# Placing the heads' products one product earlier in each step of a fused attention and mixture-of-experts kernel

## What is computed

```python
# q, k, v: (8, 8, 576, 64), float32: batch, heads, sequence, head dimension
kv = np.einsum('bhsd,bhse->bhde', k, v)
out = np.einsum('bhsd,bhde->bhse', q, kv)
rms = np.sqrt(np.mean(out * out, axis=-1, keepdims=True) + 1e-06)
x = out / rms * g_norm            # then laid out as 4608 tokens x 512

gate = 1.0 / (1.0 + np.exp(-(x @ w_gate)))   # 512 x 1536
x = gate * (x @ w_val) @ w_out               # 1536 x 512

h = x @ w_in                                 # 512 x 2048
g = where(h >= 1, h, where(h <= -1, 0, (h + 1) ** 2 / 4))
y = g @ w_out                                # 2048 x 512
```

## Time and profile before

| | |
|---|---|
| median of three runs | 1758.91 us (1757.97 to 1762.51) |
| the profiled execution, its own time | 1760.77 us |
| its span, from first to last instruction | 1759.0 us |
| TensorE matmul busy | 1680.4 us (96%) |
| VectorE busy | 1215.1 us (69%) |
| ScalarE busy | 886.3 us (50%) |
| GpSimd busy | 227.4 us (13%) |
| mean granted TensorE clock | 0.981 |

### The profile page before, as it was taken

The page is one execution under the profiler, slowest core; times in us unless marked ns, Lnnn a source line. Parts: engine busy times, 40 slices in busy tenths (PEclk is TensorE's granted clock), DMA queues, the critical chain, the costliest instruction groups (busy, mean ns, idle before and its releaser), DMA issues. The chain is left out here.

```text
span 1759.0 us, 31916 instructions
## 1 busy us (share of the span) xinstructions
PE 1680.4 (96%) x12552; PEld 1641.2 (93%) x12552; DVE 1215.1 (69%) x1725; ACT 886.3 (50%) x1612; POOL 227.4 (13%) x293
## 2 busy tenths in 40 slices
PE   8999999999879999899999899999995799999999
PEld 5799999999879999899999899999995799999999
DVE  4567677678657775787778777777773576667764
ACT  5556666655435554444445455555552344444443
POOL 3510000014333442100002500000001100000000
PEclk9999999999989999999999999999997999999999
DMA  7444443333777788944533423333338944434440
GB/s 255 136 144 132 143 145 128 104 127 126 196 198 217 211 238 258 301 142 147 151 131 137 142 104 129 130 130 130 135 135 276 304 140 128 125 120 145 143 121 37
DMA packets 229316, 278.90 MB, mean 159 GB/s; under 512 B 33072, under 2 KB 172848, under 8 KB 229168
## 3 DMA queue, kind: packets, MB, share of 16 engines
q1 hardware_dynamic: 191568, 207.66, 36.0%
q0 software_dynamic: 37600, 69.22, 13.4%
HBM read 156.76 MB, written 120.06 MB: 157 GB/s over the span
## 5 line engine op out<-in xcount | busy, mean ns | idle before, releaser
L1500 PE MATMUL x<-t_hi,v_lo 128*128 128x288 f32 x1664 | 501.3, 301 | 34.7 <-ACT kept L877 19.0
L1501 PE MATMUL x<-t_lo,v_hi 128*128 128x288 f32 x1664 | 495.2, 298 | 0.0
L1502 PE MATMUL x<-t_hi,v_hi 128*128 128x288 f32 x1664 | 494.0, 297 | 0.0
L1500 PEld LDWEIGHTS x<-t_hi,v_lo 128*128 128x128 f32 x1664 | 316.1, 190 | 42.1 <-ACT kept L877 21.2
L1502 PEld LDWEIGHTS x<-t_hi,v_hi 128*128 128x128 f32 x1664 | 317.3, 191 | 0.0
L1501 PEld LDWEIGHTS x<-t_lo,v_hi 128*128 128x128 f32 x1664 | 316.7, 190 | 0.1
L1500 PE MATMUL y<-t_hi,v_lo 128*128 128x288 f32 x832 | 250.9, 302 | 26.3 <-DVE c_tile L1054 19.6
L1501 PE MATMUL y<-t_lo,v_hi 128*128 128x288 f32 x832 | 247.5, 297 | 0.0
L1502 PE MATMUL y<-t_hi,v_hi 128*128 128x288 f32 x832 | 246.7, 296 | 0.0
L1500 PEld LDWEIGHTS y<-t_hi,v_lo 128*128 128x128 f32 x832 | 158.1, 190 | 32.5 <-DVE c_tile L1054 20.0
L1500 PE MATMUL x<-v_hi,t_lo 128*128 128x256 f32 x576 | 164.2, 285 | 8.7 <-ACT o_kept L1021 8.7
(11 more groups left out here) (195 smaller groups left out, 3647.4 us busy)
## 6 DMA issues: line engine op xcount, KB each, us to landing
g_scratch<-c_tile SPq DMA_DIRECT2D x128, 288.0 KB, 2.4
gq<-g_scratch SPq DMA_DIRECT2D x64, 512.0 KB, 6.2
h_scratch<-gate SPq DMA_DIRECT2D x192, 144.0 KB, 2.1
hq<-h_scratch SPq DMA_DIRECT2D x32, 864.0 KB, 5.1
stage<-w_in POOLq DMA_DIRECT2D x68, 256.0 KB, 3.3
kv_ring<-kv_in SPq DMA_DIRECT2D x30, 512.0 KB, 4.4
fold_hi<-fold_hi POOLq DMA_DIRECT2D x14, 896.0 KB, 5.4
fold_lo<-stage POOLq DMA_DIRECT2D x14, 896.0 KB, 7.4
```

The costliest lines, as they stand in the source:

```text
L1500: nc.tensor.matmul(dst, s_lo, m_hi, start=start, stop=False, skip_group_check=True)
L1501: nc.tensor.matmul(dst, s_hi, m_lo, start=False, stop=False, skip_group_check=True)
L1502: return nc.tensor.matmul(dst, s_hi, m_hi, start=False, stop=stop, skip_group_check=True)
```

## The change

The call of `heads` inside `attention` is made at P4's place in place of P6's. `attention(k, 4)` is called behind P4 of step k - 1, which stands directly ahead of P6 of step k, so the six matmuls of the heads move ahead of the six matmuls of P6 in 24 steps. Nothing else differs.

```diff
             def attention(k, number):
 
                 b, s = divmod(k, A_SETS)
-                if number == 6 and heads_of(k):
+                if number == 4 and heads_of(k):
                     heads(*heads_of(k))
```

## The result

| | before | after |
|---|---|---|
| median | 1759.06 us | 1777.75 us (1776.40 to 1780.12, four runs) |
| span of the profiled execution | 1759.0 us | 1776.8 us |
| TensorE matmul busy | 1680.4 us (96%) | 1684.9 us (95%) |
| VectorE busy | 1215.1 us | 1213.2 us |
| ScalarE busy | 886.3 us | 882.8 us |

The ratio is 1.0104, with a 95% interval of 1.0086 to 1.0123: 18 us slower, where 1777.0 was forecast. No engine has more work; TensorE waits.

A forecast was written before the change was run, and what follows sets the result against it. TensorE was taken to bound the heads' stretch. Five regular groups, 16.1 us, with the first group made 18.1; added to the 1758.91 median this gave 1777.0 us, own range 1774 to 1780, 8-in-10 range 1767 to 1781.

The forecast's parts named there:

- TensorE alone bounds the stretch: Over 85 to 370 us TensorE is busy 283.61 of 285.00 us, so every new wait adds its full length.
- The squares hang on P6, not on the heads: On ScalarE the squares follow P6's copy and the casts back to back, so moving P6 back delays them.
- the first rival: Only what was already late counts, so the mean square's new wait is absent: 8 to 9 us, 1767.5; chance 0.13.
- 0.72 at s = 5: In steps with two casts, TensorE's mean square waits 0.72 us for `ps_lo`, which was 0.08 early before.
- 0.62 for the heads at s = 0: At s = 0 the heads can start at 7.45 for a place at 6.83, waiting 0.62 us for `pq_lo`.
- A regular group 3.2: Each of five regular groups of four heads steps loses 3.2 us in waits and restarts, 16.1 in all.
- 0 at k = 4 in the first group: The heads fill P6's 0.91 wait, but a weight chunk's low part holds the next P1: 0, largest gain 0.8.
- What stays hidden: P7, P4, P6 and P3 still get the copies and `c` they need before their places, so no wait there.
- The longer-chain rival: Lateness of `pq_lo` reaches into the next step's cast: 4.2 to 4.5 us a group, 1783 to 1785; chance 0.09.
- The rule on VectorE's drain: If each next VectorE operation awaited an empty pipe, five distances grow 0.08, about 1.1 us a group; forecast went by rows instead.
- Not given back: Later passes just start later; the rival, chance 0.05, had the loss recovered at 470 to 480 us's folded-weight wait: 1758.9.
- the prediction's own signs of being wrong: A ScalarE gap between the casts and `ps_hi`, no wait of the mean square, or shorter passes behind.

The follow-up runs named there:

- The half at s = 4 and 5: Against the kernel before, the heads move ahead of P6 only at s = 4 and 5 (12 of 24 steps): 1766.63 us, ratio 1.0048.
- the half at s = 5 and 1: Against the kernel before, the heads move ahead of P6 only at s = 5 and s = 1: 1764.93 us, ratio 1.0024.
- the rearranged kernel: The change plus squares and high part ahead of ScalarE's copy behind P6, and `pq_lo` and `ps_lo` earlier on VectorE: 1762.80 us, 1.0022 against the kernel before.

## Why the prediction was right

By its own steps:

- *TensorE alone bounds the stretch, so every new wait counts in full.* Right: 18.3 us inside, 17.8 on the span, 18 by the ratio.
- *The squares hang on P6, not on the heads.* Right, and the point on which the first rival fell. The half at s = 4 and 5, the half at s = 5 and 1, and the squares moved ahead on ScalarE each gave what this predicts to within 0.2 us inside. The rival's 8 to 9 us for the whole change would have been 1767.5.
- *0.72 at s = 5.* Measured, from the group shown: the heads start at 195.12 and the mean square at 200.66, 5.54 later, less 4.79 for the heads, P6, P3, P2, P7 and P1: 0.75.
- *0.62 for the heads at s = 0.* From the mean square (200.66) to the heads (203.40) 2.74, less the 2.12 of the earlier trace rows: 0.62.
- *A regular group 3.2.* Measured, from group to group: 50.39 less 47.13, 3.26. Five groups and what the first has behind its first mean square make 18.3; expected were 5 x 3.2 and 2.0, 18.1.
- *0 at k = 4 in the first group.* Right. This step lies ahead of the first mean square and so outside the inside distance, and the executions differed by then: at its very first loads TensorE had waited 1.36 us in the kernel after and 0.62 in the kernel before. From a matmul of `x` that both traces show behind a short wait ahead of k = 4 (69.10 before, 70.19 after) to the first mean square (91.13 and 92.22) it is 22.03 us in both. The first heads wait 0.42 for `pq_lo`, P6 no longer waits its 0.91, and the next P1 waits 0.73 for the low part of a weight chunk (0.25 before).
- *What stays hidden.* Right: no wait for the copies behind P1, P6 or P7 has appeared in the stretch.
- *The longer-chain rival.* It fell: a group cost 3.26, not 4.2 to 4.5.
- *The rule on VectorE's drain.* The instructions behind `ps_lo` followed one another as in the earlier trace rows, 0.68, 0.37 and 0.67 apart. The prediction says that such rows contradict the Trainium skill ("VectorE: DVE Perf Modes", The DRAIN you can't avoid); that is too strong, since the same paragraph goes on: "A next op that is not held starts earlier". Both kinds stand in the traces: at s = 4 of the rearranged kernel `c` started only 0.03 behind the end of `pq_lo`, in all six groups, and cost the 0.1 a group named above. There it is the first instruction to read PSUM behind the copies of `kv_raw`, which take half of the partitions each; directly behind these copies it had also started 0.03 behind the end in the kernel before. Whether that is the cause was not tested.
- *Not given back.* Right in the main: the execution ends 17.8 us later, and of the 18.3 nothing came back where the rival had it, at the waits for folded weights. Over 265 us from 460 (before) and from 480 (after) TensorE waited 17.9 and 20.9 us for ScalarE's copy of line 877, which stands there behind casts of folded weights; in the four experiments with that line it was 17.4 to 19.3. But one of the prediction's own signs of being wrong, passes behind that are shorter than before, did appear: from the last mean square to the end it was 1759.0 - 348.2 = 1410.8 us and is 1776.8 - 367.6 = 1409.2. The sign was badly chosen, since this distance lies between 1405.6 and 1410.8 in the eight profiled executions, and the kernel before has the longest of them. The 17.8 of the spans is near 18.3 in part by chance: the start had added 1.1 and the passes behind took 1.6 away, as told in the last section.
- *How the waits would show.* I expected 16 or 17 waits of the mean square and about 6 us; the profile lists 13 and 6.9. The waits of 0.14 are not listed; the 13 are the first mean square's and one behind each s = 5 and s = 0.

## What to carry to other kernels

When work moves within the list of the engine that bounds, look on the other engines not for who uses its result, but for what stands ahead of that user in its list: here the squares could start only behind a copy that the move had pushed back, and an input that had come 0.08 us early came 0.72 late. Move the followers' lists together with it, or leave it. And judge a wait by taking away its cause: to move only the instruction that waits shifts the same lateness to the next place that needs the chain.

## What the runs showed beside this

In the profiled executions the clock behind a wait far from the change was not the same each time. Behind the end of the second product, TensorE waited 2.80 us in the kernel before and 1.87 in the one after (the wait of line 1009), and in six microseconds that begin 2.2 to 2.5 us behind it the granted clock was 0.74 and 1.00. The windows of the kernel before:

```profile
1016.00:1022.00 6.00, 6.00 (x36) 6.00 (x36) 4.10 (x7) 2.81 (x5) 0.00 (x0) 0.74 0.27 101
```

and of the kernel after:

```profile
1036.00:1042.00 6.00, 6.00 (x48) 6.00 (x47) 5.31 (x8) 3.32 (x7) 0.00 (x0) 1.00 0.26 101
```

48 matmuls in place of 36 in the same six microseconds: the lower level (1.2 GHz in place of 2.4) cost the kernel before about 1.6 us there (12 matmuls at 0.13), and its longer wait another 0.9. A start that was 19.4 us late at the last mean square (18.3 and 1.1 from the start of the execution) and 21.1 us at the end of the second product was so 18.6 us late behind this stretch. Another 0.9 went at the wait for `c_tile` (line 1054), 18.12 us in the kernel before, near 1358 us, and 17.24 in the kernel after, near 1376 us, which leaves 17.8 at the end. The 1.7 us between 19.4 and 21.1 lie in the stretch with the waits for folded weights, which also vary. Whether the change made the wait of line 1009 shorter, or chance did, is open: it was 1.88, 2.33, 2.62, 3.01, 1.93 and 2.83 in the six experiments, in no order that follows their delays. The clock did follow the wait: it fell to 1.2 GHz for 3.4 us behind it in the four executions with 2.62 us and more, and stayed at 2.4 GHz in the four with 2.33 and less. No run changed this wait alone, so that is an observation and not a test. Effects of 2 us on the median of this kernel should therefore be read from the distances inside the stretch that an edit touches.
